# One queue for all loads, and another sequence for the first five steps of windowed attention, in a fused attention and two-feed-forward kernel

## Time and profile before

| what | us |
|---|---|
| median of 3 runs | 513.01 |
| the runs | 510.52 to 514.62 |
| profiled execution, its own time | 516.8 |
| its span | 514.9 |
| TensorE busy | 486.9 |
| VectorE busy | 267.8 |
| ScalarE busy | 254.5 |
| GpSimd busy | 94.8 |

### The profile page before, as it was taken

The page is one execution under the profiler, slowest core; times in us unless marked ns, Lnnn a source line. Parts: engine busy times, 40 slices in busy tenths (PEclk is TensorE's granted clock), DMA queues, the critical chain, the costliest instruction groups (busy, mean ns, idle before and its releaser), DMA issues.

```text
span 514.9 us, 9377 instructions
## 1 busy us (share of the span) xinstructions
PE 486.9 (95%) x3784; PEld 436.4 (85%) x3784; DVE 267.8 (52%) x482; ACT 254.5 (49%) x665; POOL 94.8 (18%) x159
## 2 busy tenths in 40 slices
PE   3668979999999999999999999999999999999997
PEld 2458969878888888877899979989998899989997
DVE  2539986497547946396349644834044503440040
ACT  2865865486538755486058474335213621262212
POOL 3638312241232221241003110001000100020000
PEclk9979979999999999999999999999999999999999
DMA  8961225201430312005000500001100010002002
GB/s 253 375 211 34 72 59 179 72 0 42 144 103 2 101 44 83 1 0 205 1 1 3 193 5 1 0 1 47 46 1 2 24 69 1 0 1 93 1 0 93
DMA packets 24223, 33.03 MB, mean 64 GB/s; under 512 B 1522, under 2 KB 13810, under 8 KB 24180
## 3 DMA queue, kind: packets, MB, share of 16 engines
q1 hardware_dynamic: 22324, 29.01, 17.1%
q10 hardware_dynamic: 1856, 3.42, 1.8%
HBM read 27.71 MB, written 4.72 MB: 63 GB/s over the span
## 4 chain that ended last, share of the span: by engine, by line
PE 82%; DVE 6%; DMA 4%; issue 3%; ACT 3%; POOL 1%; SPq 0%; ACTq 0%; DVEq 0%; POOLq 0%
PE dense L391 38%; PE pt_ps L391 10%; PE score L391 9%; PE pt_ps L586 6%; PE score L586 6%; DMA qk<-q_t 4%; PE x_ps L391 4%; PE x_ps L453 3%; PE pt_ps L437 3%; PE score L423 2%; DVE tmp L889 2%; DVE wr L874 1%; ACT vp L638 1%; PE score L416 1%; DVE ar L902 1%
## 5 line engine op out<-in xcount | busy, mean ns | idle before, releaser
L391 PE MATMUL dense<-xr,wr 128*128 128x512 f32 (+2 forms) x480 | 101.4, 371 | 3.3 <-POOL wr L1117 1.7
L391 PEld LDWEIGHTS dense<-xr,wr 128*128 128x128 f32 x480 | 87.8, 188 | 16.2 <-POOL wr L1117 2.0
L391 PE MATMUL dense<-ar,wr 128*128 128x512 f32 (+2 forms) x456 | 99.3, 374 | 0.3 <-DVE wr L874 0.3
L391 PEld LDWEIGHTS dense<-ar,wr 128*128 128x128 f32 x456 | 82.4, 188 | 11.5 <-DVE wr L874 0.6
L889 DVE SCALAR_TENSOR_TENSOR tmp<-tmp,taps 128x512 f32<-128x512 f32 (+2 forms) x80 | 57.7, 722 | 22.2 <-ACT tmp L679 20.7
L1111 POOL TENSOR_TENSOR vp<-vp,recip 128x1024 f32<-128x1024 f32 x18 | 34.5, 1917 | 108.3 <-DVE recip L853 108.3
L638 ACT ACTIVATE vp<-score,bias 128x128 f32<-128x128 f32 x128 | 45.0, 382 | 1.3 <-PE pt_ps L437 0.6
L1188 POOL TENSOR_TENSOR ident<-ident,minus_half 128x1 f32<-128x1 f32 (+1 forms) x20 | 11.0, 548 | 155.5 <-DVE ident L997 155.5
L671 ACT ACTIVATE tmp<-dense 128x512 f32<-128x512 f32 (+2 forms) x40 | 21.9, 549 | 34.0 <-PE dense L391 34.0
L805 ACT ACTIVATE ar<-vp 128x576 fp32r<-128x576 f32 x16 | 11.0, 687 | 50.1 <-DVE vp L1047 50.1
L391 PE MATMUL dense<-wr,xr 128*128 128x512 f32 x144 | 33.3, 389 | 0.0
(11 more groups left out here) (97 smaller groups left out, 752.2 us busy)
## 6 DMA issues: line engine op xcount, KB each, us to landing
vp<-v_rows SPq DMA_DIRECT2D x36, 256.0 KB, 4.0
out_t<-vp SPq DMA_DIRECT2D x16, 288.0 KB, 2.1
qk<-k_t SPq DMA_DIRECT2D x9, 384.0 KB, 3.8
qk<-q_t SPq DMA_DIRECT2D x9, 384.0 KB, 5.5
x2keep<-w_in ACTq DMA_DIRECT2D x2, 1024.0 KB, 11.0
qk<-w_in SPq DMA_DIRECT2D x1, 2048.0 KB, 9.6
x2keep<-w_out ACTq DMA_DIRECT2D x1, 1280.0 KB, 11.3
vp<-w_spatial_t SPq DMA_DIRECT2D x1, 1152.0 KB
```

The lines of the kernel that those rows point to most:

```text
L391: last = mm(dst, stationary(a, t), moving(c, t), start=(t == 0 and n == 0), stop=(t == of - 1 and n == 2))
```

## The change

The edits, engine by engine:

- **SP** issues all loads of the first stage. Batch 0 of k and q comes in four parts (columns 0 to 127, to 255, to 383, to 575), with a semaphore of its own for the last. The order is: three parts, v 0 and 1, the first half of w_in, the fourth part, the taps, then after scores 1 the first third of batch 1, v 2 and 3, the second half of w_in; after values 0, v 4 and 5 and then five tiles of w_out.
- **TensorE**: scores 4 move behind transposes 2 (they were ahead of values 1), and scores 3 wait for the fourth part of k and q. The pieces of chunk 0 go 6, 8, 9, 9 over the doubles instead of 13, 6, 5, 8. In the last cycle (chunk 3, double 16), 5 of the 11 pieces come ahead of transposes 17 instead of behind.
- **ScalarE** issues no loads. split_in 2 to 5 stand behind x_high 1, split_in 6 and 7 behind x_high 2, and exponentials 4 behind them. split_out 0 to 3 move into `up(0)`, one behind each of tiles f = 3 to 6.
- **VectorE**: reciprocals 3 stand ahead of x_low 1, maximum 4 behind copy_transposed 2, reciprocals 4 behind copy_transposed 3. out_low 0 and 1 move into `up(0)` behind f = 6 and 7, out_low 2 takes the place of 4 in double 3, and 3 to 7 stand behind double 5's reciprocals.
- **GpSimd**: in_low 2 to 7 all stand between normalise 3 and normalise 4.

```diff
--- before.py
+++ after.py
@@ -165,6 +165,7 @@
         qk_first = sem("qk_first")
         qk_second = sem("qk_second")
         qk_rest = sem("qk_rest")
+        qk_last = sem("qk_last")
         qk_third = [sem(f"qk_third{i}") for i in range(3)]
         v_loaded = [sem(f"v_loaded{i}") for i in range(4)]
         in_loaded = [sem(f"in_loaded{i}") for i in range(2)]
@@ -240,7 +241,6 @@
 
         RAMP = NEED[0]
         CYCLES = [list(range(NEED[c], NEED[c + 1])) for c in range(NC - 1)]
-        K_MID = 4 * WINDOW
         THIRD = S // 3
 
         def window(j):
@@ -275,7 +275,7 @@
 
 
         PIECES = [(d, t) for t in range(FT) for d in range(KT - 1)] + [(KT - 1, t) for t in range(FT)]
-        SHARES = [[13, 6, 5, 8], [13, 6, 5, 8], [13, 6, 5, 8], [13, 11, 8]]
+        SHARES = [[6, 8, 9, 9], [13, 6, 5, 8], [13, 6, 5, 8], [13, 11, 8]]
         assert all(sum(s) == len(PIECES) and len(s) == len(y) for s, y in zip(SHARES, CYCLES))
 
         N_PIECES = WI // 512
@@ -327,14 +327,29 @@
                 sp.dma_start(k_sb[:, :, cols], k[b, :, :, cols]).then_inc(qk_third[r], 16)
                 sp.dma_start(q_sb[:, :, cols], q[b, :, :, cols]).then_inc(qk_third[r], 16)
 
-            for cols, loaded in ((slice(0, P), qk_first), (slice(P, K_MID), qk_second), (slice(K_MID, S), qk_rest)):
-                sp.dma_start(k_sb[:, :, cols], k[0, :, :, cols]).then_inc(loaded, 16)
-                sp.dma_start(q_sb[:, :, cols], q[0, :, :, cols]).then_inc(loaded, 16)
-            for g in range(4):
-                load_v(g)
+            def load_first(lo, hi, loaded):
+                sp.dma_start(k_sb[:, :, lo:hi], k[0, :, :, lo:hi]).then_inc(loaded, 16)
+                sp.dma_start(q_sb[:, :, lo:hi], q[0, :, :, lo:hi]).then_inc(loaded, 16)
+
+
+            w_in_t = w_in.rearrange("(t p) n -> p t n", p=P)
+            w_out_t = w_out.rearrange("(t p) n -> p t n", p=P)
+            load_first(0, P, qk_first)
+            load_first(P, 2 * P, qk_second)
+            load_first(2 * P, 3 * P, qk_rest)
+            load_v(0)
+            load_v(1)
+            sp.dma_start(raw_in[:, :, 0:F // 2], w_in_t[:, :, 0:F // 2]).then_inc(in_loaded[0], 16)
+            load_first(3 * P, S, qk_last)
+            sp.dma_start(taps[:, :], conv_w).then_inc(taps_loaded, 16)
+            sp.wait_ge(score_done, 2)
+            load_third(1, 0)
+            load_v(2)
+            load_v(3)
+            sp.dma_start(raw_in[:, :, F // 2:F], w_in_t[:, :, F // 2:F]).then_inc(in_loaded[1], 16)
 
             last_reader = (3, 6, 8)
-            for n in range(-1, DOUBLES):
+            for n in range(DOUBLES):
                 for b in range(1, B):
                     for r in range(3):
                         if (NB * (b - 1) + last_reader[r]) // 2 == n + 2:
@@ -346,11 +361,12 @@
                     sp.wait_ge(pv_done, n + 1)
                     for g in (2 * n + 4, 2 * n + 5):
                         load_v(g)
+                if n == 0:
+                    sp.dma_start(raw_out_a, w_out_t[:, 0:OUT_A, :]).then_inc(out_loaded[0], 16)
                 if n == RAMP - 1:
 
                     sp.wait_ge(split_lo_in, N_PIECES)
-                    sp.dma_start(raw_out_b, w_out.rearrange("(t p) n -> p t n", p=P)[:, OUT_A:FT, :]
-                                 ).then_inc(out_loaded[1], 16)
+                    sp.dma_start(raw_out_b, w_out_t[:, OUT_A:FT, :]).then_inc(out_loaded[1], 16)
 
             sp.wait_ge(score_done, DOUBLES)
             sp.dma_start(raw_in2, w_in2.rearrange("(t p) n -> p t n", p=P)).then_inc(in2_loaded, 16)
@@ -395,8 +411,8 @@
             def scores(n):
                 s = score_view(n)
                 steps = [divmod(g, NB) for g in (2 * n, 2 * n + 1)]
-                if n < 3:
-                    pe.wait_ge((qk_first, qk_second, qk_rest)[n], 32)
+                if n < 4:
+                    pe.wait_ge((qk_first, qk_second, qk_rest, qk_last)[n], 32)
                 for b, j in steps:
                     if b and j % 3 == 0:
                         pe.wait_ge(qk_third[j // 3], 32 * b)
@@ -509,11 +525,14 @@
             scores(1)
             scores(2)
             transposes(0)
-            for n in range(RAMP):
-                if n + 3 < RAMP + 2:
-                    scores(n + 3)
-                values(n)
-                transposes(n + 1)
+            scores(3)
+            values(0)
+            transposes(1)
+            values(1)
+            transposes(2)
+            scores(4)
+            values(2)
+            transposes(3)
             for c in range(NC - 1):
                 up(c)
                 done = 0
@@ -521,9 +540,13 @@
                     if n + 2 < DOUBLES:
                         scores(n + 2)
                     values(n)
+
+                    early = 0 if n + 2 < DOUBLES or n + 1 == DOUBLES else share // 2
+                    for i in range(done, done + early):
+                        down_piece(c, i)
                     if n + 1 < DOUBLES:
                         transposes(n + 1)
-                    for i in range(done, done + share):
+                    for i in range(done + early, done + share):
                         down_piece(c, i)
                     done += share
             up(NC - 1)
@@ -692,32 +715,23 @@
                         act.wait_ge(gated_done, n + 1)
                         nc.scalar.activation(gated[0][:, f - 2, 0:W], conv[:, n % 4, 0:W], ACT.Copy
                                              ).then_inc(gated_hi, 1)
-
-            w_in_t = w_in.rearrange("(t p) n -> p t n", p=P)
-            w_out_t = w_out.rearrange("(t p) n -> p t n", p=P)
-            act.wait_ge(qk_second, 32)
-            act.dma_start(raw_in[:, :, 0:F // 2], w_in_t[:, :, 0:F // 2]).then_inc(in_loaded[0], 16)
-            act.dma_start(taps[:, :], conv_w).then_inc(taps_loaded, 16)
+                    if c == 0 and 3 <= f < 7:
+                        split_out(f - 3)
+
             exponentials(0)
-            act.dma_start(raw_in[:, :, F // 2:F], w_in_t[:, :, F // 2:F]).then_inc(in_loaded[1], 16)
             exponentials(1)
-            for i in range(0, 2):
-                split_in(i)
-            act.dma_start(raw_out_a, w_out_t[:, 0:OUT_A, :]).then_inc(out_loaded[0], 16)
+            split_in(0)
+            split_in(1)
             exponentials(2)
-            for i in range(2, 4):
-                split_in(i)
             x_high(0)
             exponentials(3)
-            for i in range(4, 6):
+            x_high(1)
+            for i in range(2, 6):
                 split_in(i)
-            x_high(1)
-            exponentials(4)
+            x_high(2)
             for i in range(6, 8):
                 split_in(i)
-            x_high(2)
-            for t in range(0, 4):
-                split_out(t)
+            exponentials(4)
 
             act.wait_ge(taps_loaded, 16)
             act.wait_ge(zero_cols, 1)
@@ -901,6 +915,8 @@
                         dve.wait_ge(gated_hi, n + 1)
                         vec.tensor_tensor(gated[1][:, f - 2, 0:W], conv[:, n % 4, 0:W],
                                           gated[0][:, f - 2, 0:W].bitcast(F32), ALU.subtract).then_inc(gated_lo, 1)
+                    if c == 0 and f in (6, 7):
+                        out_low(f - 6)
 
             def keep_x2(c, d):
 
@@ -920,15 +936,17 @@
             softmax_maximum(2)
             reciprocals(1)
             copy_transposed(0)
-            for n in range(RAMP):
-                if n + 3 < RAMP + 2:
-                    softmax_maximum(n + 3)
-                    reciprocals(n + 2)
-                x_low(n)
-                copy_transposed(n + 1)
-            reciprocals(RAMP + 1)
-            for t in range(0, 4):
-                out_low(t)
+            softmax_maximum(3)
+            reciprocals(2)
+            x_low(0)
+            copy_transposed(1)
+            reciprocals(3)
+            x_low(1)
+            copy_transposed(2)
+            softmax_maximum(4)
+            x_low(2)
+            copy_transposed(3)
+            reciprocals(4)
 
             dve.wait_ge(zero_cols, 1)
             for c in range(NC - 1):
@@ -940,7 +958,7 @@
                     if n + 2 < DOUBLES:
                         softmax_maximum(n + 2)
                     if n == RAMP:
-                        out_low(4)
+                        out_low(2)
                     x_low(n)
                     if n + 1 < DOUBLES:
                         copy_transposed(n + 1)
@@ -950,7 +968,7 @@
                     if n + 2 < DOUBLES:
                         reciprocals(n + 2)
                     if n == RAMP:
-                        for t in range(5, FT):
+                        for t in range(3, FT):
                             out_low(t)
                 keep_x2(c, KT - 1)
             up(NC - 1)
@@ -1155,11 +1173,9 @@
             normalise(2)
             in_low(1)
             normalise(3)
-            in_low(2)
-            in_low(3)
+            for i in range(2, N_PIECES):
+                in_low(i)
```

(2 more changed lines are left out.)

## The result

| | kernel before | changed kernel |
|---|---|---|
| runs | 16 | 16 |
| median, us | 513.67 | 508.62 |
| lowest to highest, us | 510.52 to 515.58 | 508.00 to 510.75 |
| profiled execution, us | 516.8 | 508.95 |
| its span, us | 514.9 | 507.2 |

The ratio of the runs is 0.9905, with a 95% interval of 0.9889 to 0.9922. The forecast was 506 in a range of 501 to 511, and 509.8 for the profiled execution. The second figure is off by 0.9 us, the first by 2.6: between the two profiled executions the gain is 7.9 us, between the medians 5.05. Where these 2.8 us lie is the first question of the experiments.

The account below looks back on a forecast made before the run. The prediction took TensorE's idle and slow time in the ramp (first 71 us) as the bound. Ramp 5.8 plus last cycle 1.2 gave 7.0 us: 509.8 profiled, 506 on the median, range 501 to 511.

Parts of the forecast that it names:

- Loads: First loads: with one queue, scores 4 no longer wait for a transfer; the old wait was 5.6 us.
- The walk to `up(0)`: First doubles: `up(0)` starts at 30.2 us instead of 38.01, and the 1.7 us stall on GpSimd goes.
- Inside `up(0)`: Taps begin at 34.4 us instead of 45.59, ScalarE's round is 2.48; scores 6 at 60.4 instead of 70.67.
- Scores 7: Behind five out_low on VectorE: 71.2 us instead of 79.71; five pieces (2.7 us) come later, net ramp gain 5.8.
- Transposes 17: Last cycle: five pieces ahead of them cover the 1.2 us wait for normalise 17; gain 1.2 us.
- The sum: 5.8 + 1.2 = 7.0 us: profiled execution 516.8 to 509.8, then 506 on the median by an edge of 3.8.
- the first rival: Gain sinks in and behind `up(0)` (4.5 of 7.0 us), or the median's wait was smaller: 510.5 us; chance 0.26.
- The second rival: TensorE at 1.2 GHz from scores 3 to mid `up(0)`: 7 us slower, 520 on the median; chance 0.09.

Follow-up runs that it names:

- w_out as before: Changed kernel with split_out 0 to 3 and out_low 0 to 3 back ahead of `up(0)` and pieces 13, 6, 5, 8: 505.18 us.
- early pieces alone: Kernel before with one edit, 5 of the 11 pieces of double 16 ahead of transposes 17 in the last cycle: 512.71 us.
- loads and early pieces: Kernel before with the change's loads and the 5 pieces ahead of transposes 17, all other sequences as before: 508.04 us.
- loads alone: Kernel before with the change's loads only (one queue, fourth part of k and q, w_out behind values 0): 509.43 us.

## Why the prediction was right, point by point

**Loads.** Right. Scores 4 waited for nothing, q's third took 7.5 us instead of 16. By the Trainium skill (DMA: Bandwidth & Descriptors, "Queues, rings and completion order") each engine takes turns between the queues that have work. The traces agree: with w_in in a second queue q's third took 12.5 to 16.1 us (four traces), in one queue 7.5 to 9.0 (ten). The runs change the queue and the order of the loads together, so they don't show which of the two does it. What I had not seen is that `up(0)` still is a draw: the first part of q can come 0.6 us late (5.87 against 5.25).

**The walk to `up(0)`.** 29.93 against 30.2. It was right for partly wrong reasons. I took both kernels as alike up to 19.5 us. In fact ScalarE's table load, free of the transfers ahead of it, moved to the very start, and transposes 0 came 1 us sooner; a half clock from 15 to 20 us took that back (scores 3 end at 19.42 in both kernels, values 0 start at 19.35). And in_low took 1.25 us each and not 1.67, so that x_low 2 released `up(0)` and not in_low 3, which the walk had at 30.2. The granted clock was 1.00 from 21 to 50 us, as the prediction wanted from 20.

**Inside `up(0)`.** Taps at 34.18 (34.4 predicted), ScalarE's round 2.46 (2.48). Maximum 5 at 55.38, 0.8 later than the walk: the slow first taps held the first sigmoid by 0.4 us, where I had added nothing for them, and both out_low lay on the path, not one. Scores 6 at 61.21 against 60.4.

**Scores 7.** 70.65 against 71.2. The walk's own terms add up to 71.0 (66.7 + 1.4 + 2.9). The term was mis-sized: five out_low at 1.21 us each, 6.0; they took 4.75. The three of the earlier trace rows were one pass of 2.42, beside normalise, and two of 0.68. A mean over a group was the wrong price for five.

**Transposes 17.** 1.2 us, and it was.

**The sum.** 7.0 predicted, 7.9 found between the profiled executions. The failed step is the last one, from 509.8 to 506: "That lay 3.8 above the median of the runs; the same edge below gives 506". The edge was not an offset common to both kernels. Most of it was the longer transfer wait of that one execution, which the change removes, and 0.7 of it came from a median of three runs (513.01; 16 runs give 513.67, and an edge of 3.1); the changed kernel's profiled execution lies 0.3 us from its median (0.6 in its second trace). In the first rival I had named that the median's wait may be smaller, and left it out of the figure. 5.6 us of wait were in one trace; 2.0 in another.

**Rivals.** 508.6 lies about halfway between the forecast's 506 and the first rival's 510.5, but not by its mechanism: between the profiled executions 7.9 us were gained, so nothing of the forecast sank in `up(0)` or behind it. What came true is its last clause, that the median run had less of the wait to lose. For the chances that decides: a gain of 0.95%, interval 0.78 to 1.11, sits at the bound of 1%, just on the side to which I gave 0.26 and not 0.65. That the forecast of 509.8 for the profile held is in part luck, for one cost of the change was not seen. Against w_out as before, the stretch from taps to maximum is 3.9 us longer: 2.0 by the insertions, where I counted 1.0, and 1.9 by the slow first taps. This did not show in the forecast since I compared with the kernel before, which had slow taps as well and out_low ahead of them. The second rival did not come: the half clock was there, but only from 15 to 20 us.

## What to carry to other kernels

One trace is one draw: where a wait for a transfer is on the path and two queues share the engines, take a second trace before pricing it, and don't carry the distance between a profiled execution and the median over to the new kernel. And where an edit acts late, measure from an event just ahead of it: of 2.9 us between two traces, 1.4 were there before the edit did anything. Fill the idle time ahead of a known wait with work that is ready: here a first portion of 6 pieces instead of 9 cost 1.5 us or more. Work put into a loop that two engines run in step is not free: four splits and two out_low, 3.6 us in full, cost it 2.0. And what an engine does sooner, it does beside other work: the taps began 2.8 us sooner than in w_out as before, beside GpSimd, and were done later.

## What the hardware did that I had not expected

**One pass of VectorE can take 3.6 times as long beside one of GpSimd.** out_low takes 0.68 us, and 2.42 when it meets normalise (1.90 us long), while a maximum, which reads PSUM, is not slowed (1.22 us at 63.02, beside the same normalise). The Trainium skill (SBUF — State Buffer, "Who interferes with whom") says that a VectorE instruction with two inputs in SBUF contends with a GpSimd instruction that reads SBUF, since its second input comes through the read interface that the two share, and it calls the shared ports an exclusive lock. The traces agree: 2.42 is close to 1.90 and 0.68 together.

**Ahead of scores 6, an idle time of 1.9 us left the clock at full and one of 3.0 never did.** Scores 6 and the values and transposes behind them ran at full clock (0.41 us for the first four matmuls) behind 1.94 and behind 0.38 us of idle time; behind 5.48 scores 6 ran at the half (0.64). Behind 2.98 they were slow at once in four traces (the kernel before, early pieces alone, loads and early pieces, w_out as before); in the second trace of the kernel before and in that of the loads alone the first four still took 0.41, but the clock was at half by the values behind them (1.98 and 1.97 us instead of 1.15). TensorE had run `up(0)` and the first pieces ahead of them in all of these. It is no rule for other places: in the ramp of w_out as before, where TensorE had only short groups to run, the clock fell behind an idle time of 1.96 us: work began again at 21.67, and 0.64 was granted from 22 to 23 us and 0.50 from 23 to 25.

**ScalarE's table load moved to the start.** No edit was made for that. With no transfers to issue ahead of its first exponential, and no wait for q and k ahead of these, the load of the table stood at 0.72 us of the span and not at 9.41, and transposes 0 came 1 us sooner. Before and after:

```profile
...
9.41 1.28 ACT L638 ACT_TABLE_LOAD   x1 [9.41 <-issue]
...
```

```profile
...
0.72 1.28 ACT L661 ACT_TABLE_LOAD   x1 [0.72 <-PEq L1235]
...
```

The other runs bear it out: 9.41 to 9.55 in the four traces with the old loads, the changed sequence with old loads among them (9.47), and 0.72 or 0.73 in the ten with the new ones.
